# Bit projections in two products instead of three, and bits by comparing two halves

## The chip, the cores and the metric

The kernel runs on one core of a Trainium2 chip. The metric is the device time of one execution in microseconds (us). The kernel is written with explicit semaphores: every engine has its own program, runs it in order and waits where a semaphore says so.

## What is computed

Attention with a bucket mask, then a top-1 mixture of eight experts, then a dense layer pair. The change touches the first part alone, where each query and key gets six bits, one for each column of `proj`; a query may look at a key only if all six agree.

```python
batch, n_heads, seq, head_dim = (2, 8, 768, 64)      # 16 heads; proj is 64 x 6
q_bits = (np.einsum('bhsd,dk->bhsk', q, proj) > 0).astype(np.int64)
k_bits = (np.einsum('bhsd,dk->bhsk', k, proj) > 0).astype(np.int64)
powers = 2 ** np.arange(n_bits)
q_bucket = np.sum(q_bits * powers, axis=-1)
k_bucket = np.sum(k_bits * powers, axis=-1)
mask = q_bucket[:, :, :, None] == k_bucket[:, :, None, :]
scores = scale * np.matmul(q, k.transpose(0, 1, 3, 2))
scores = np.where(mask, scores, -1000000000.0)
...
attn = attn / (np.sum(attn, axis=-1, keepdims=True) + 1e-09)
return np.matmul(attn, v).astype(np.float32)
```

The sign of a projection has to be right for values near zero, so it is not enough to multiply in a reduced format. The kernel splits a number into a high part (rounded to `fp32r`) and a low part (the rest) and adds the products high x high, low weight x high input, and high weight x low input.

## The kernel before

**Stages.** The first 270 us are attention over 16 heads, then come routing (some 15 us), the experts and the dense layers. The experts' stage starts when the last head's rows are written.

**A head.** A head g has two sides, c = 0 (queries) and c = 1 (keys); `u = 2g + c` counts them. Each side holds 768 tokens as 128 partitions x 384 columns: two tokens' 64 dimensions lie above each other, so that partitions 0 to 63 and 64 to 127 hold different tokens. For a side:

- `turn_qk` (TensorE) transposes the raw rows into a bank of PSUM, `bank_a`.
- `split_hi` (ScalarE, lines 595 and 597) copies the bank out as the high part; `split_lo` (VectorE, line 767) makes the low part `x_lo`.
- `project` (TensorE, line 1097) forms three products of 384 columns in the same bank.
- `sign` (VectorE, line 783) makes `bits`, 1.0 where the projection is positive.
- `code` (TensorE, line 1105) multiplies the bits by a pattern matrix, so that all 64 buckets stand in a row each; `mask_even` (VectorE, line 791) and `mask_odd` (ScalarE, lines 605 and 608) turn this into one-hot rows, `q_a` and `k_a`, that the score products add.

GpSimd copies the parts to their places (lines 465 to 496).

**Groups.** The order on each engine is written by hand. A head is three groups (`part` 0, 1, 2), and a group n works on two score tiles of 128 queries. On TensorE a group holds the scores of tiles m_s and m_s + 1 (`pair_s`, `pair_t`, line 1119, eight products), the transposes of earlier exponentials (`turn_exps`, line 1130), and, by part, pieces of an earlier head's product with v (`times_v`, line 1146) and output product (`last`, line 1157), and of the next head's preparation. On VectorE a group holds `copy_t1` (line 799, transposed exponentials out of PSUM) and `row_max` (line 775); on ScalarE `copy_t0` (line 627), `exp_rows` (line 618), `copy_u` (line 634) and `copy_rows`.

**Waits.** Scores of tile m wait for the exp of tile m - 2. `code` waits for `sign`, `turn_qk` of a side waits for both masks of the side before, and `exp_rows` waits for `row_max`. `bank_a` is used by all sides except head 0's keys.

Of the kernel before, what the change touches and what calls it, by code (L numbers as in the profile page):

```python
# [22 lines left out]
ALU = mybir.AluOpType  # L23
ACT = mybir.ActivationFunctionType
AX = mybir.AxisListType
F32 = mybir.dt.float32
F32R = mybir.dt.float32r
# [4 lines left out]
P = 128  # L32
# [4 lines left out]
B, H, S, D = 2, 8, 768, 64  # L37
NBITS = 6
BUCKETS = 2 ** NBITS
HEADS = B * H  # L40
# [15 lines left out]
HALF = S // 2  # L56
# [70 lines left out]
def program(nc, q, k, v, proj, w_gate, w_ogate, w1, w2, w_in, w_out, const, out):  # L127
    with ExitStack() as ctx:
        sem = lambda n: ctx.enter_context(nc.semaphore(n))
# [30 lines left out]
        with ExitStack() as att:  # L160
            sb = lambda n, s, d=F32: att.enter_context(nc.sbuf_tensor(n, s, d))
            sb("w_first", [P, 2, SET])
            v_nat = sb("v_nat", [P, 4, J, D])
            exps = sb("exps", [P, 4, S])
            exps_t = sb("exps_t", [P, J, S])
            den = sb("den", [P, 4, J])
            rows_sb = sb("rows_sb", [P, 2, J, QE])
            u_sb = sb("u_sb", [P, S])
            last_w = sb("last_w", [P, H, QE])
            raw = sb("raw", [P, 2, 2, J, D])  # L170
            q_a = sb("q_a", [P, 2, S], F32R)
            k_a = sb("k_a", [P, 2, S], F32R)
            q_b = sb("q_b", [P, 2, S], F32R)
            k_b = sb("k_b", [P, 2, S], F32R)
            x_lo = sb("x_lo", [P, 2, HALF], F32R)
            bits = sb("bits", [P, 2, HALF], BF16)
            nmax = sb("nmax", [P, 2, J])
            proj2 = sb("proj2", [P, NBITS])
            pat = sb("pat", [P, P])
            pat_bf = sb("pat_bf", [P, P], BF16)  # L180
            proj_w = sb("proj_w", [P, 2, P], F32R)


        with ExitStack() as rt:
# [78 lines left out]
        prep_bank = lambda u: bank_b if u == 1 else bank_a  # L263
# [17 lines left out]
        s_pat = sem("s_pat")  # L281
        s_bits = sem("s_bits")
        s_sgn = sem("s_sgn")
        s_code = sem("s_code")
        s_mq, s_mk = sem("s_mq"), sem("s_mk")
        s_sc = sem("s_sc")
        s_mx = sem("s_mx")
# [300 lines left out]
        def _(act):  # L588
# [10 lines left out]
            def mask_odd(g, c):  # L599
# [7 lines left out]
                else:  # L607
                    act.activation(tiles(k_a, g, 1)[D:P], turned(prep_bank(u))[D:P], ACT.Relu, scale=BIG,
                                   bias=unmatched[D:P, :]).then_inc(s_mk, 1)

            def exp_rows(m):
                g, qt = m // J, m % J
                act.wait_ge(s_mx, m + 1)
                if g >= 4 and qt == 0:
                    act.wait_ge(s_x, g - 3)
                if m >= 4:
                    act.wait_ge(s_pt, 2 * (m - 3))
                act.activation(exps[:, m % 4, :].rearrange("p (h n) -> p h n", h=2), score_pair[m % 2][:, :, 0:HALF],  # L618
                               ACT.Exp, bias=nmax[:, g % 2, qt:qt + 1],
                               accum_out=den[:, g % 4, qt:qt + 1]).then_inc(s_ex, 1)  # L620

            def copy_t0(m):
                g, qt = m // J, m % J
                if g >= 1:
                    act.wait_ge(s_av, 2 * (g - 1) + qt // 3 + 1)
                act.wait_ge(s_pt, 2 * m + 1)
                act.activation(exps_t[:, 0:JH, qt * P:(qt + 1) * P],  # L627
                               pair_u[:, 0, 0:HALF].rearrange("p (j n) -> p j n", j=JH), ACT.Copy).then_inc(s_t0, 1)

            def copy_u(g, h):  # L630
                act.wait_ge(s_av, 2 * g + h + 1)
                if g >= 1:
                    act.wait_ge(s_fin, g)
                act.activation(u_sb[:, h * HALF:(h + 1) * HALF], bank_b[:, 0:HALF], ACT.Copy).then_inc(s_u, 1)  # L634
# [36 lines left out]
            for n in range(3, GROUPS):  # L671
                g, part = n // 3, n % 3
                m_s, m_e = 2 * (n - GROUP_S), 2 * (n - GROUP_E)
                if 0 <= m_e - 1 < J * HEADS - 1:
                    copy_t0(m_e - 1)
                if part == 0 and 3 <= g < HEADS + 2:
                    copy_rows(g - 3)
                if g < HEADS and part == 1:
                    split_hi(g, 1)
                if g < HEADS and part == 2:  # L680
                    mask_odd(g, 1)
                if 0 <= m_e < J * HEADS:
                    copy_t0(m_e)
                if m_s < J * HEADS:
                    exp_rows(m_s)
                    exp_rows(m_s + 1)
                if n == 3 * HEADS + 3:
                    copy_t0(m_e + 1)
                if g >= 2 and part <= 1:
                    copy_u(g - 2, part)  # L690
                if g < HEADS and part == 0:
                    mask_odd(g, 0)
                if g + 1 < HEADS and part == 2:
                    split_hi(g + 1, 0)
# [53 lines left out]
        def _(dve):  # L748
# [11 lines left out]
            def split_lo(g, c):  # L760
                u = 2 * g + c
                if u >= 2:
                    dve.wait_ge(s_cp, copies(u - 2))
                    dve.wait_ge(s_bits, u - 1)
                dve.wait_ge(s_hi, u + 1)
                hi = tiles(k_b, g, 1) if c else tiles(q_b, g, 0)
                dve.scalar_tensor_tensor(turned(x_lo[:, c, :]), turned(prep_bank(u)), SCALE if c else 1.0,
                                         hi.bitcast(F32), ALU.mult, ALU.subtract).then_inc(s_lo, 1)
# [9 lines left out]
            def sign(g, c):  # L778
                u = 2 * g + c
                if u >= 2:  # L780
                    dve.wait_ge(s_code, u - 1)
                dve.wait_ge(s_bits, u + 1)
                dve.tensor_scalar(bits[:, c, :], prep_bank(u)[:, 0:HALF], 0.0, None, ALU.is_gt).then_inc(s_sgn, 1)

            def mask_even(g, c):
                u = 2 * g + c
# [7 lines left out]
            def copy_t1(m):  # L794
                g, qt = m // J, m % J
                if g >= 1:
                    dve.wait_ge(s_av, 2 * (g - 1) + qt // 3 + 1)
                dve.wait_ge(s_pt, 2 * m + 2)
                dve.tensor_copy(exps_t[:, JH:J, qt * P:(qt + 1) * P],  # L799
                                pair_u[:, 1, 0:HALF].rearrange("p (j n) -> p j n", j=JH)).then_inc(s_t1, 1)  # L800
# [23 lines left out]
            for n in range(3, GROUPS):  # L824
                g, part = n // 3, n % 3
                m_s, m_e = 2 * (n - GROUP_S), 2 * (n - GROUP_E)
                if 0 <= m_e - 1 < J * HEADS:
                    copy_t1(m_e - 1)
                if g < HEADS and part == 0:
                    split_lo(g, 0)  # L830
                if m_s < J * HEADS:
                    row_max(m_s)
                if g < HEADS and part == 2:
                    mask_even(g, 1)
                if m_s < J * HEADS:
                    row_max(m_s + 1)
                if g < HEADS and part == 0:
                    sign(g, 0)
                if g < HEADS and part == 1:
                    split_lo(g, 1)  # L840
                if 0 <= m_e < J * HEADS:
                    copy_t1(m_e)
                if g < HEADS and part == 0:
                    mask_even(g, 0)
                if n == 3:
                    dve.wait_ge(s_cst, 16)
                    dve.tensor_copy(last_w[:, :, 0:D],
                                    cc("twice").unsqueeze(1).broadcast_to([P, H, D])).then_inc(s_setup, 1)
                if n == 9:
                    dve.tensor_copy(tri_bf[:, :], cc("tri"))  # L850
                    dve.tensor_copy(ones_bf[:, :], cc("ones"))
                    dve.tensor_copy(iota_bf[:, :], cc("iota"))
                if part == 1 and g >= 2:
                    inverse(g - 2)
                if part == 1 and 8 <= g < 8 + NCH:
                    dve.wait_ge(s_wld[g - 8], 16)
                    dve.tensor_copy(chunk_of(w_part, 0, 0, g - 8), w_raw[0][g - 8][:, :]).then_inc(s_whi, 1)
                if g < HEADS and part == 1:
                    sign(g, 1)
# [216 lines left out]
        def _(pe):  # L1076
# [13 lines left out]
            def project(g, c):  # L1090
                u = 2 * g + c
                hi, lo = (tiles(k_b, g, 1) if c else tiles(q_b, g, 0)), x_lo[:, c, :]
                pe.wait_ge(s_lo, u + 1)
                if u == 0:
                    pe.wait_ge(s_setup, 1)
                for n, (w, x) in enumerate(((0, hi), (1, hi), (0, lo))):
                    mm = pe.matmul(prep_bank(u)[:, 0:HALF], proj_w[:, w, :], x, start=n == 0, stop=n == 2)  # L1097
                mm.then_inc(s_bits, 1)

            def code(g, c):  # L1100
# [293 lines left out]
```

## Time and profile before

| | |
|---|---|
| median of 3 runs | 800.01 us (799.96 to 800.34) |
| profiled execution | 799.7 us |
| its span, first to last instruction | 797.9 us |
| mean granted TensorE clock | 0.999 |
| TensorE (PE) busy | 780.0 us |
| TensorE weight loads (PEld) busy | 657.8 us |
| VectorE (DVE) busy | 454.9 us |
| ScalarE (ACT) busy | 361.7 us |
| GpSimd (POOL) busy | 339.2 us |

The profile is that of one execution. Matmuls are pipelined and their recorded ends are modelled, so the spacing of their starts is a better measure than their length. The chain is followed back from the last instruction, at each step to what released it.

### The profile page before, as it was taken

What the parts mean: (1) busy time and instruction counts of PE and PEld (TensorE: products, weight loads), DVE (VectorE), ACT (ScalarE), POOL (GpSimd) and SP (SyncE); (2) the same over time, 40 slices, a digit from 0 to 9 for tenths busy, and PEclk for the clock granted to TensorE, in tenths of its full rate; (3) what the DMA queues carried; (4) which work ended last, traced back from release to release, by engine and by line L of the source; (5) the groups of instructions that cost most, each with busy time, mean ns of one, the idle gap of its engine ahead of it and who ended that gap; (6) DMA issues with size and microseconds to landing.
All of it is one profiled execution on the core that took longest, in us unless ns stands there. A gap on an engine that the chain in (4) does not pass through costs nothing.

```text
span 797.9 us, 12941 instructions
## 1 busy us (share of the span) xinstructions
PE 780.0 (98%) x4389; PEld 657.8 (82%) x4389; DVE 454.9 (57%) x801; ACT 361.7 (45%) x684; POOL 339.2 (43%) x333
## 2 busy tenths in 40 slices
PE   7999999999999889999999999999999999999997
PEld 5777787778777578888888888899889889989985
DVE  6787778788877574544445445559427416613720
ACT  5777777677766322344322440057117305603610
POOL 4244434565554179977779883125210020000000
PEclk9999999999999999999999999999999999999999
DMA  6222322121100086775656750440010020000000
GB/s 174 80 70 74 101 89 67 50 71 41 41 21 12 21 278 227 248 235 175 196 175 228 239 166 27 155 137 1 26 53 2 1 67 14 0 14 28 1 14 26
DMA packets 40942, 72.68 MB, mean 91 GB/s; under 512 B 17904, under 2 KB 24304, under 8 KB 40880
## 3 DMA queue, kind: packets, MB, share of 16 engines
q10 hardware_dynamic: 9520, 31.60, 12.2%
q1 hardware_dynamic: 27920, 28.98, 11.6%
q0 software_dynamic: 3440, 11.28, 4.3%
q8 instruction: 39, 0.64, 0.3%
q14 instruction: 23, 0.19, 0.1%
HBM read 60.56 MB, written 11.28 MB: 90 GB/s over the span
## 4 chain that ended last, share of the span: by engine, by line
PE 63%; issue 28%; DVE 4%; POOL 2%; ACT 2%; DMA 0%; POOLq 0%; DVEq 0%; ACTq 0%
PE pair_s L1266 13%; PE pair_t L1281 13%; PE bank_b L1146 8%; PE pair_u L1130 8%; PE pair_s L1119 4%; PE pair_t L1119 4%; PE bank_b L1157 2%; PE bank_a L1097 2%; PE pair_u L1245 2%; PE bank_a L1086 1%; POOL out L567 1%; PE pair_s L1318 1%; DVE g_lo L1066 1%; PE bank_a L1105 1%; POOL y_raw L561 1%
## 5 line engine op out<-in xcount | busy, mean ns | idle before, releaser
L436 POOL TENSOR_TENSOR w_part<-w_raw,w_part 128x1024 fp32r<-128x1024 f32 x80 | 190.1, 2405 | 57.5 <-ACT w_part L658 56.8
L658 ACT ACTIVATE w_part<-w_raw 128x1024 fp32r<-128x1024 f32 x72 | 73.9, 1055 | 135.8 <-PE pair_t L1281 102.9
L1368 PE MATMUL pair_t<-w_part,g_hi 128*128 128x512 f32 x384 | 119.0, 391 | 0.3 <-POOL w_part L436 0.3
L1266 PE MATMUL pair_s<-w_part,xs_t 128*128 x456 | 108.8, 394 | 0.4 <-DVE xs_t L944 0.4
L1281 PE MATMUL pair_t<-w_part,hid_t 128*128 x456 | 109.0, 394 | 0.0
L567 POOL DMA_INDIRECT out<-o_sb,token x12 | 11.8, 984 | 208.5 <-DVE o_sb L1036 208.5
L1266 PEld LDWEIGHTS pair_s<-w_part,xs_t 128*128 128x128 f32 x456 | 84.2, 188 | 17.8 <-issue 0.9
L1281 PEld LDWEIGHTS pair_t<-w_part,hid_t 128*128 128x128 f32 x456 | 84.4, 188 | 16.8
L734 ACT ACTIVATE elu<-elu 128x384 f32<-128x384 f32 x64 | 33.6, 524 | 121.2 <-DVE elu L1056 121.1
L1368 PEld LDWEIGHTS pair_t<-w_part,g_hi 128*128 128x128 f32 x384 | 71.6, 188 | 15.2 <-issue 0.7
L1130 PE MATMUL pair_u<-first,exps 128*128 128x128 f32 x576 | 79.2, 273 | 1.5 <-ACT exps_t L627 1.0
L1368 PE MATMUL pair_t<-w_part,g_lo 128*128 128x512 f32 x192 | 74.9, 390 | 0.0
L1130 PEld LDWEIGHTS pair_u<-first,exps 128*128 128x128 f32 x576 | 67.4, 141 | 5.4 <-ACT exps L618 2.0
L1146 PE MATMUL bank_b<-exps_t,v_nat 128*64 128x384 f32 x384 | 69.0, 494 | 0.7 <-ACT u_sb L634 0.7
L1318 PE MATMUL pair_u<-y_t,w_part 128*128 128x384 f32 x384 | 69.3, 334 | 0.3 <-DVE elu L1061 0.3
L1318 PE MATMUL pair_s<-y_t,w_part 128*128 128x384 f32 x384 | 69.3, 335 | 0.0
L1318 PEld LDWEIGHTS pair_u<-y_t,w_part 128*128 128x128 f32 x384 | 66.8, 188 | 0.7 <-DVE elu L1061 0.6
L1318 PEld LDWEIGHTS pair_s<-y_t,w_part 128*128 128x128 f32 x384 | 66.9, 188 | 0.2
L799 DVE COPY exps_t<-pair_u 128x384 f32<-128x384 f32 x96 | 53.1, 553 | 20.4 <-PE pair_u L1130 18.7
L962 DVE CAST hid_t<-pair_u 128x512 fp32r<-128x512 f32 x38 | 26.1, 686 | 67.2 <-PE pair_u L1245 67.2
L627 ACT ACTIVATE exps_t<-pair_u 128x384 f32<-128x384 f32 x96 | 47.2, 491 | 21.0 <-PE pair_u L1130 20.1
L953 DVE TENSOR_SCALAR hid<-pair_s 128x1024 f32<-128x1024 f32 x19 | 23.3, 1225 | 46.8 <-PE pair_s L1266 46.8
(196 smaller groups left out, 1234.9 us busy)
## 6 DMA issues: line engine op xcount, KB each, us to landing
w_raw<-in_moe_w ACTq DMA_DIRECT2D x48, 512.0 KB, 6.2
w_raw<-in_moe_w SPq DMA_DIRECT2D x16, 512.0 KB, 5.0
ys_sorted<-ys SPq DMA_DIRECT2D x19, 256.5 KB, 3.5
w_raw<-in_moe_w_in ACTq DMA_DIRECT2D x8, 512.0 KB, 6.6
raw<-in_q SPq DMA_DIRECT2D x16, 192.0 KB, 2.4
raw<-in_k SPq DMA_DIRECT2D x16, 192.0 KB, 2.6
v_nat<-in_v SPq DMA_DIRECT2D x16, 192.0 KB, 2.3
x_rows<-rows_sb SPq DMA_DIRECT2D x16, 192.0 KB, 2.3
```

The source lines that it names most:

```text
L436: pool.tensor_tensor(chunk_of(w_part, n, 1, c), w_raw[n % 2][c][:, :], chunk_of(w_part, n, 0, c).bitcast(F32), ALU.subtract).then_inc(s_wl ...
L627: act.activation(exps_t[:, 0:JH, qt * P:(qt + 1) * P], pair_u[:, 0, 0:HALF].rearrange("p (j n) -> p j n", j=JH), ACT.Copy).then_inc(s_t0, 1)
L658: act.activation(chunk_of(w_part, n, 0, c), w_raw[n % 2][c][:, :], ACT.Copy).then_inc(s_whi, 1)
L734: act.activation(elu[:, n % 3, :], elu[:, n % 3, :], ACT.Exp).then_inc(s_em, 1)
L799: dve.tensor_copy(exps_t[:, JH:J, qt * P:(qt + 1) * P], pair_u[:, 1, 0:HALF].rearrange("p (j n) -> p j n", j=JH)).then_inc(s_t1, 1)
L1119: mm = pe.matmul(score_pair[m % 2][:, h, 0:HALF], a[:, g % 2, t], b[:, g % 2, h * HALF:(h + 1) * HALF], start=first, stop=not first)
L1130: mm = pe.transpose(pair_u[:, part, n * P:(n + 1) * P], exps[:, m % 4, kt * P:(kt + 1) * P], ident)
L1146: mm = pe.matmul(bank_b[o * D:(o + 1) * D, 0:HALF], v_nat[:, g % 4, 2 * i + o, :], exps_t[:, 2 * i + o, h * HALF:(h + 1) * HALF], start=i ...
L1266: mm = pe.matmul(pair_s[:, h, :], xs_t[:, xp, c * P:(c + 1) * P], w_part[:, bass.ds(par, 1), wp, a:a + 512], start=c == 0 and xp == 0 and ...
L1281: mm = pe.matmul(pair_t[:, s % 2, :], hid_t[:, hp, c * P:(c + 1) * P], w_part[:, bass.ds(par, 1), wp, a:a + DM], start=c == 0 and n == 0, ...
L1318: mm = pe.matmul(hidden_bank[n % 4][:, 0:NB], w_in_p[:, wp, c, f * P:(f + 1) * P], y_t[:, yp, c, :], start=c == 0 and m == 0, stop=c == CD ...
L1368: mm = pe.matmul(pair_t[:, t % 2, :], gp[:, f, j * P:(j + 1) * P], w_out_p[:, wp, f, :], start=f == 0 and m == 0, stop=f == FT - 1 and m == 2)
```

## The change

From head 1 on a side's projection has two products. A third block of the weight operand, `proj_w[:, 2, :]`, has the high weights in columns 0 to 63 and the low weights in columns 64 to 127. One product with the high input gives high x high on the output's partitions 0 to 63 and low x high on 64 to 127; the second product, high weights with the low input, adds to partitions 0 to 63. The projection is the sum of the two halves, which no instruction forms: ScalarE copies the upper half to `low_sb` (`keep_low`), and VectorE writes a bit where minus the lower half is smaller than that copy. Head 0 stays as it was. The third block is built in group 3 by two VectorE copies, and TensorE waits for them at u = 2. `sign` of the query side moves behind `copy_t1` in VectorE's order.

```diff
-            proj_w = sb("proj_w", [P, 2, P], F32R)
+            proj_w = sb("proj_w", [P, 3, P], F32R)
+            low_sb = sb("low_sb", [P, 2, HALF])
...
+            def keep_low(g, c):
+                u = 2 * g + c
+                act.wait_ge(s_sgn, u - 1)
+                act.wait_ge(s_bits, u + 1)
+                act.activation(low_sb[0:D, c, :], prep_bank(u)[D:P, 0:HALF], ACT.Copy).then_inc(s_low, 1)
...
                 if 0 <= m_e < J * HEADS:
                     copy_t0(m_e)
+                if g < HEADS and part == 0:
+                    keep_low(g, 0)
                 if m_s < J * HEADS:
                     exp_rows(m_s)
                     exp_rows(m_s + 1)
...
                 if g >= 2 and part <= 1:
                     copy_u(g - 2, part)
+                if g < HEADS and part == 1:
+                    keep_low(g, 1)
...
-                dve.wait_ge(s_bits, u + 1)
-                dve.tensor_scalar(bits[:, c, :], prep_bank(u)[:, 0:HALF], 0.0, None, ALU.is_gt).then_inc(s_sgn, 1)
+                if g == 0:
+                    dve.wait_ge(s_bits, u + 1)
+                    dve.tensor_scalar(bits[:, c, :], prep_bank(u)[:, 0:HALF], 0.0, None, ALU.is_gt).then_inc(s_sgn, 1)
+                else:
+                    dve.wait_ge(s_low, u - 1)
+                    dve.scalar_tensor_tensor(bits[0:D, c, :], prep_bank(u)[0:D, 0:HALF], -1.0, low_sb[0:D, c, :],
+                                             ALU.mult, ALU.is_lt).then_inc(s_sgn, 1)
...
+                if n == 3:
+                    dve.wait_ge(s_setup, 1)
+                    for w in range(2):
+                        done = dve.tensor_copy(proj_w[:, 2, w * D:(w + 1) * D], proj_w[:, w, 0:D].bitcast(F32))
+                    done.then_inc(s_both, 1)
...
-                if g < HEADS and part == 0:
-                    sign(g, 0)
                 if g < HEADS and part == 1:
                     split_lo(g, 1)
                 if 0 <= m_e < J * HEADS:
                     copy_t1(m_e)
+                if g < HEADS and part == 0:
+                    sign(g, 0)
...
-                for n, (w, x) in enumerate(((0, hi), (1, hi), (0, lo))):
-                    mm = pe.matmul(prep_bank(u)[:, 0:HALF], proj_w[:, w, :], x, start=n == 0, stop=n == 2)
+                if u == 2:
+                    pe.wait_ge(s_both, 1)
+                parts = ((0, hi), (1, hi), (0, lo)) if g == 0 else ((2, hi), (0, lo))
+                for n, (w, x) in enumerate(parts):
+                    mm = pe.matmul(prep_bank(u)[:, 0:HALF], proj_w[:, w, :], x, start=n == 0, stop=n == len(parts) - 1)
```

On VectorE the query side of a steady head stood so before; `bits` is `sign`, `q_a` is `mask_even`, and the second row of `exps_t` belongs to the next group:

```order
L767 SCALAR_TENSOR_TENSOR x_lo<-bank_a,q_b 128x384
L775 TENSOR_REDUCE nmax<-pair_s 128x1
L775 TENSOR_REDUCE nmax<-pair_t 128x1
L783 TENSOR_SCALAR bits<-bank_a 128x384
L799 COPY exps_t<-pair_u 128x3x128
L791 TENSOR_SCALAR q_a<-bank_a,first 64x3x128
L799 COPY exps_t<-pair_u 128x3x128
```

And so in the changed kernel, with its own line numbers:

```order
L780 SCALAR_TENSOR_TENSOR x_lo<-bank_a,q_b 128x384
L788 TENSOR_REDUCE nmax<-pair_s 128x1
L788 TENSOR_REDUCE nmax<-pair_t 128x1
L817 COPY exps_t<-pair_u 128x3x128
L800 SCALAR_TENSOR_TENSOR bits<-bank_a,low_sb 64x384
L809 TENSOR_SCALAR q_a<-bank_a,first 64x3x128
L817 COPY exps_t<-pair_u 128x3x128
```

`sign` changed places with `copy_t1` and has a second operand. On ScalarE, the same stretch and the next group before; `u_sb` is `copy_u`, `rows_sb` is `copy_rows`:

```order
L642 ACTIVATE rows_sb<-bank_b 128x480
L627 ACTIVATE exps_t<-pair_u 128x3x128
L618 ACTIVATE exps,den<-pair_s,nmax 128x768
L618 ACTIVATE exps,den<-pair_t,nmax 128x768
L634 ACTIVATE u_sb<-bank_b 128x384
L605 ACTIVATE q_a<-bank_a,first 64x3x128
L627 ACTIVATE exps_t<-pair_u 128x3x128
L597 ACTIVATE k_b<-bank_a 128x3x128
L627 ACTIVATE exps_t<-pair_u 128x3x128
L618 ACTIVATE exps,den<-pair_s,nmax 128x768
L618 ACTIVATE exps,den<-pair_t,nmax 128x768
L634 ACTIVATE u_sb<-bank_b 128x384
```

And in the changed kernel:

```order
L651 ACTIVATE rows_sb<-bank_b 128x480
L636 ACTIVATE exps_t<-pair_u 128x3x128
L618 ACTIVATE low_sb<-bank_a 64x384
L627 ACTIVATE exps,den<-pair_s,nmax 128x768
L627 ACTIVATE exps,den<-pair_t,nmax 128x768
L643 ACTIVATE u_sb<-bank_b 128x384
L608 ACTIVATE q_a<-bank_a,first 64x3x128
L636 ACTIVATE exps_t<-pair_u 128x3x128
L600 ACTIVATE k_b<-bank_a 128x3x128
L636 ACTIVATE exps_t<-pair_u 128x3x128
L627 ACTIVATE exps,den<-pair_s,nmax 128x768
L627 ACTIVATE exps,den<-pair_t,nmax 128x768
```

One copy to `low_sb` stands ahead of the two exps of part 0; the one of the key side comes behind the `u_sb` of part 1, one row further on.

## Rows read from the trace of the kernel before

**Rows 1.** The page, part 1: busy time of each engine.
```profile
PE 780.0 (98%) x4389; PEld 657.8 (82%) x4389; DVE 454.9 (57%) x801; ACT 361.7 (45%) x684; POOL 339.2 (43%) x333
```

**Rows 2.** Windows, attention stage: PE, PEld, DVE, ACT, POOL busy, clock, DMA.
```profile
20.00:260.00 240.00, 239.31 (x1643) 188.33 (x1642) 187.64 (x309) 173.51 (x373) 112.16 (x188) 1.00 0.21 60
```

**Rows 3.** Chain that ended last, one head: start, us, what.
```profile
119.55 0.70 PE pair_s L1119 x4
...
121.60 0.53 PE bank_a L1097 x3
...
124.22 0.27 PE bank_a L1105
...
125.14 0.70 PE pair_s L1119 x4
...
129.63 0.73 PE bank_a L1097 x3
...
132.43 0.18 PE bank_a L1105
...
135.55 0.70 PE pair_s L1119 x4
```

**Rows 4.** Groups by form on TensorE, 23 to 246 us: busy, mean ns.
```profile
L1097 PE MATMUL bank_a<-x_lo,proj_w 128*128 128x384 f32 x28 | 9.4, 337 | 0.0
```

**Rows 5.** Timeline of ScalarE, the same head: start, us.
```profile
121.76 0.90 ACT L618 ACTIVATE exps<-pair_s,nmax 128x768 f32<-128x768 f32 x1
...
122.64 0.90 ACT L618 ACTIVATE exps<-pair_t,nmax 128x768 f32<-128x768 f32 x1
...
124.26 0.49 ACT L634 ACTIVATE u_sb<-bank_b 128x384 f32<-128x384 f32 x1 [0.64 <-PE bank_b L1146]
124.78 0.57 ACT L605 ACTIVATE q_a<-bank_a,first 64x384 fp32r<-64x384 f32 x1
...
129.68 0.49 ACT L634 ACTIVATE u_sb<-bank_b 128x384 f32<-128x384 f32 x1
130.79 0.49 ACT L627 ACTIVATE exps_t<-pair_u 128x384 f32<-128x384 f32 x1 [0.62 <-PE pair_u L1130]
...
134.71 0.89 ACT L618 ACTIVATE exps<-pair_t,nmax 128x768 f32<-128x768 f32 x1
```

**Rows 6.** Timeline of VectorE, the same head.
```profile
120.21 0.56 DVE L767 SCALAR_TENSOR_TENSOR x_lo<-bank_a,q_b 128x384 fp32r<-128x384 f32 x1
...
121.55 0.95 DVE L775 TENSOR_REDUCE nmax<-pair_t 128x1 f32<-128x768 f32 x1
122.42 0.55 DVE L783 TENSOR_SCALAR bits<-bank_a 128x384 bf16<-128x384 f32 x1
122.88 0.55 DVE L799 COPY exps_t<-pair_u 128x384 f32<-128x384 f32 x1
...
130.47 0.56 DVE L783 TENSOR_SCALAR bits<-bank_a 128x384 bf16<-128x384 f32 x1 [0.66 <-PE bank_a L1097]
...
133.39 0.96 DVE L775 TENSOR_REDUCE nmax<-pair_t 128x1 f32<-128x768 f32 x1
```

**Rows 7.** Timeline of TensorE at the start; in brackets idle time and releaser.
```profile
14.10 0.34 PE L1105 MATMUL bank_a<-bits,pat_bf 128*128 128x384 bf16 x1 [1.41 <-DVE bits L783]
...
17.80 0.63 PE L1097 MATMUL bank_a<-k_b,proj_w 128*128 128x384 f32 x2 [0.88 <-DVE x_lo L767]
...
21.70 0.52 PE L1086 MATMUL bank_a<-first,raw 128*128 128x128 f32 x3 [0.21 <-DVE k_a L791]
```

**Rows 8.** Timeline of VectorE at the start.
```profile
13.50 0.55 DVE L783 TENSOR_SCALAR bits<-bank_a 128x384 bf16<-128x384 f32 x1
...
18.71 0.56 DVE L783 TENSOR_SCALAR bits<-bank_a 128x384 bf16<-128x384 f32 x1 [0.50 <-PE bank_a L1097]
...
20.98 0.61 DVE L791 TENSOR_SCALAR k_a<-bank_a,first 64x384 fp32r<-64x384 f32 x1
```

**Rows 9.** Timeline of ScalarE at the start, the fourth exp's accumulator.
```profile
18.87 0.20 ACT L618 ACTIVATION_READ_ACCUMULATOR exps<-pair_t,nmax 128x1 f32 x1
```

More of the change, by code:

```diff
@@ L283, in program @@
         s_sgn = sem("s_sgn")
+        s_low = sem("s_low")
         s_code = sem("s_code")
+        s_both = sem("s_both")
         s_mq, s_mk = sem("s_mq"), sem("s_mk")
```

## The prediction

> **What bounds the kernel now.** I read the page first, then the windows, then the chain, then the timelines of the engines around the edit, and last the first 24 us, where the edit also puts new waits.
>
> On the page the reader is to see TensorE busy for 98% of the span [rows 1]. Busy time of pipelined matmuls can flatter, so the windows come next: in the 240 us from 20 to 260, the attention stage, TensorE has 239.31 us, at a granted clock of 1.00, its upper level of 2.4 GHz [rows 2]. The decisive view is the chain that ended last [rows 3]. Through one head it holds nothing but TensorE pieces, one behind another: scores at 119.55 and again at 135.55 are the same place in two neighbouring heads, so a head costs 16.00 us. So in the steady heads an instruction taken off TensorE is worth its full spacing, until something else comes late. The attention stage is followed by routing and the experts, which start when the last head is done, so what is won there is handed on.
>
> **The change, part by part.**
>
> *The removed product.* A projection of head 1 or later has two products instead of three. The chain gives three products in 0.53 us for the q side [rows 3], 0.177 each. The k side takes 0.73, the same three plus 0.20 ahead of the first one, which follows the 64-column products of times_v; that 0.20 stays, since a first product stays. There are 28 such projections between 23 and 246 us, that is 14 heads with two sides each: the 28 `x_lo` products of [rows 4], one for each. 28 x 0.176 = 4.9 us, if nothing comes late.
>
> The Trainium skill, page "TensorE: Matmul & The Clock Gate", section "Back-to-back issue gap", gives a warm isolated gap of N/2.4 + 2.5 ns, an estimate of 162.5 ns at 384 columns, by which the removed products would be worth 4.55 us. The row shows 177 and has this kernel's weight loads in it, so I stay with the row; the two differ by 0.4 us.
>
> *keep_low, the q side (steady heads).* ScalarE gets a 64x384 copy out of PSUM. No row of before is that instruction. Its nearest rows are the 128x384 copy out of PSUM, 0.49 us, and the 64x384 form with a bias, 0.57 [rows 5]; I take 0.49. When can it start? The products of head g's q side end at 122.13 by the chain (121.60 + 0.53), 0.18 earlier now: 121.95. A hand-over from TensorE costs about 0.1 (the k side ends at 129.63 + 0.73 = 130.36 [rows 3], and VectorE's bits start at 130.47 [rows 6]). So keep_low runs from 122.05 to 122.54. Behind it on ScalarE stand the two exps, which started at 121.76 and 122.64 [rows 5]: they move to about 122.5 and 123.4 and end by 124.4. Who waits for them? The scores of the next group at 125.14 on TensorE (124.96 now) [rows 3] want the first, which is done by 123.5; those 0.70 behind them want the second, done by 124.4 against 125.7. The ScalarE copy u_sb, at 124.26 [rows 5], starts at about 124.4, and its reader is the times_v of the next group, which stands behind eight score products and two turns. ScalarE then stands idle until TensorE has turned the next k side, where the 0.75 us is made up. So this costs nothing; its cover is ScalarE's waiting for TensorE before u_sb (0.64 us in [rows 5]) and over 1 us of slack at the next scores.
>
> *sign, the q side.* It moves behind copy_t1 on VectorE and becomes a scalar_tensor_tensor. The priced neighbour is x_lo, the same form from the same bank, 0.56 [rows 6], against 0.55 for the old one. VectorE's queue goes 121.55 row_max, 122.42 copy_t1, 122.88 sign, the last two having changed places [rows 6], and low_sb is there at 122.6, so the queue decides and not ScalarE. The bits are ready at 123.44. TensorE wants them for code at 124.22 [rows 3], 124.04 now. Slack 0.6 us, where there was 1.25. Cost nothing; were the chain of two engines later by x, each head would pay x - 0.6.
>
> *keep_low and sign, the k side.* The products end at 130.36 - 0.35 = 130.01. ScalarE has just finished u_sb (129.68 [rows 5], 0.18 earlier now) and used to stand idle 0.62 us before the copy at 130.79. keep_low fits in this hole: 130.12 to 130.61. VectorE's sign then runs from 130.66 to 131.21, and code wants it at 132.43 - 0.35 = 132.08 [rows 3]: slack 0.87. Against TensorE's new pace the VectorE queue behind it is some 0.35 us late, shrinking to 0.15 to 0.25 at the second row_max, which was at 133.39 and ended at 134.35 [rows 6], 0.36 before its exp at 134.71 [rows 5]. That is the thinnest margin of the steady heads: used up, but not crossed.
>
> *The start, head 1.* Here TensorE isn't full and waits for VectorE, so the same edits cost. Two 128x64 copies build the third weight part ahead of the first row_max: nothing to 0.46 us each (the spacing of 128x384 copies in [rows 6]); I take 0.25 for both, since they have a sixth of the elements each. The bits at 13.50 and TensorE's code at 14.10, which already waited 1.41 us, move by that 0.25 [rows 7, 8], so does the k side at 17.80, which waits for x_lo; it then saves 0.18. Next, head 1's k side: keep_low stands behind two exps on ScalarE, and the second's accumulator read ends at 19.07 [rows 9], 19.3 now. keep_low runs to 19.75, sign starts at 19.8 instead of 18.71 [rows 8]. Behind sign on VectorE come copy_t1 (20.26), row_max (20.72) and mask_even of k_a at 21.6, which was at 20.98 [rows 8]. For that one TensorE already waited, at 21.70 [rows 7]: it now starts at about 22.3. After this TensorE is full again. So head 1 costs +0.6 us with its two removed products already in it. Bounds: -0.35 (all hidden) and +1.1 (sign's whole lateness).
>
> The larger memset at the start lies in VectorE's first idle wait. The s_both wait is over when scores end.
>
> *The sum.* -4.9 + 0.6 = -4.3 us on the profiled execution of 799.7 (span 797.9 and 1.8 around it): 795.4. The median is 0.3 above that execution: **795.7 us**.
>
> **The rivals.**
>
> *A, new waits eat part of it.* The margins of 0.6 (q side) and 0.36 (second exp) are crossed by some tenths, for instance because a PSUM copy that starts at partition 64 and lands at 0, or the compare with an SBUF operand, is dearer than its neighbours. For it: the path now goes over two engines and two hand-overs. Against: it takes 0.6 before anything is paid. At 0.1 us a head, 14 heads give back 1.4: 797.1.
>
> *B, slower.* The mechanism is code of the q side, waiting on TensorE for sign, behind keep_low. It decides when the chain keep_low to sign is more than 0.6 + 0.35 = 0.95 us longer than worked out; at 1.2 us longer a head pays 0.6 and saves 0.35, so 14 x 0.25 + 0.6 = +4.1: 804. No row has a copy of this size above 0.6 us, so little speaks for it.
>
> *C, no change.* TensorE isn't what bounds the stage, and the removed product turns into idle time. Weight loads are busy only 188.33 of 240 us [rows 2]. Against: the chain has no piece of another engine between 119.55 and 135.55. In that case the time is 800 to 800.6 with the start's loss. The Trainium skill, page "Trainium Kernel Development and Optimization", section "Best Practices", says to judge the distance to the roofline by the weight loads' busy share and not by the matmuls'; by that 78% this stage would have room, and the rule speaks for C. It concerns the distance to the peak, while the chain tells who waits for whom, and I follow the chain.
>
> *D, the start costs nothing.* Then -4.9 - 0.35: 794.8. It is a variant of the forecast.
>
> That the edit doesn't do what it says is excluded by the instruction order: each later projection has two products.
>
> **How the numbers follow.** Forecast, D with it (794.6 to 796.6): 0.80. A (796.6 to 798.4): 0.08. C: 0.08. B: 0.04. The range reaches from D's end a little into A: 794.5 to 797.2. About 0.2%, 1.6 us, is what a measurement of this kernel tells from no change; forecast and A lie below 798.4, so faster 0.88, same 0.08, slower 0.04.
>
> **What would show it.** In the changed profile: 66 projection products where there were 96; a head of 15.65 us in the chain, still TensorE alone; ScalarE copies of 0.49; sign at 0.56 starting right behind copy_t1 on the q side; no wait of TensorE for bits in the steady heads; a wait of some 0.8 us before the first turn of head 2. The forecast is wrong if the chain shows VectorE or ScalarE pieces once a head, or if a head is shorter by much other than 0.35.

## The result

The changed kernel takes 797.95 us, median of 15 runs (797.57 to 798.88), against 799.96 us (15 runs) for the kernel before: a ratio of 0.9977, 95% interval 0.997 to 0.9984. It is 2.0 us faster; 4.3 us were forecast, and the range (794.5 to 797.2) does not hold the median. In 8 of the 15 runs the mean granted clock was 0.998 or more and the time 797.57 to 797.95; in the other 7 it was 0.995 to 0.997 and the time 798.24 to 798.88. The profiled execution is one of the 7: it took 798.58 us, with a span of 796.7 us and a mean granted clock of 0.996 where before had 0.999.

From the page, busy time of each engine, to be held against [rows 1]; 30 products and 30 weight loads fewer, 30 ScalarE copies more:

```profile
PE 778.7 (98%) x4359; PEld 654.1 (82%) x4359; DVE 451.5 (57%) x803; ACT 376.7 (47%) x714; POOL 338.9 (43%) x333
```

The chain of the changed kernel over one steady head (start, us, what), against [rows 3]:

```profile
119.62 0.33 PE bank_a L1109 x3
119.95 0.74 PE pair_u L1156 x6
...
122.76 0.35 PE bank_a L1123 x2
...
130.61 0.56 PE bank_a L1123 x2
...
135.36 0.33 PE bank_a L1109 x3
```

It is still TensorE alone, and both projections lost their product (0.53 to 0.35, 0.73 to 0.56). But the turns of the next head's query side (`bank_a L1109`), 15.74 us apart, say that a head takes 15.74 and not 15.65. The one piece that grew by more than 0.02 is the six transposes behind the turn (`pair_u L1156`): 0.74 us, where all other groups of six take 0.65 or 0.66.

Then the start. Windows of TensorE in the changed kernel: stretch, its length, busy (matmuls), granted clock, DMA share, GB/s:

```profile
10.00:15.00 5.00, 3.06 (x16) 1.00 0.41 119
15.00:20.00 5.00, 4.95 (x24) 0.66 0.21 62
```

And the timeline of TensorE there:

```profile
14.45 0.34 PE L1131 MATMUL bank_a<-bits,pat_bf 128*128 128x384 bf16 x1 [1.51 <-POOL q_b L497]
14.69 0.59 PE L1145 MATMUL pair_s<-k_a,q_a 128*128 128x384 f32 x2
15.11 0.56 PE L1145 MATMUL pair_s<-k_b,q_b 128*128 128x384 f32 x2
15.57 0.98 PE L1145 MATMUL pair_t<-k_a,q_a 128*128 128x384 f32 x2
16.35 0.84 PE L1145 MATMUL pair_t<-k_b,q_b 128*128 128x384 f32 x2
```

From about 15.4 to 18.8 us the clock was granted at its lower level, 1.2 GHz: two products that take 0.51 at 2.4 GHz take 0.84. The kernel before kept 1.00 in these windows. This fall is in the profiled execution, but not in each (below).

Two stretches of each trace hold nearly the whole account; what comes after them took 527.05 us before and 526.84 changed. The first goes from head 1's query turn to head 2's query turn (10.12 to 21.70 in the kernel before, 10.26 to 24.14 in the changed one), the second from there to the first product after the last head (270.83 and 269.89).

| | start, us | second stretch, us |
|---|---|---|
| before | 11.58 | 249.13 |
| changed | 13.88 (+2.30) | 245.75 (-3.38) |
| forecast | +0.6 | -4.9 |

### The profile page after: what moved, and what is told of

Same layout as the page of the kernel before. It is cut to its first block, busy times and chain, and to the rows that moved or that the text cites. A ratio compares the mean times of both kernels' runs of the same rounds, so it can differ in the third digit from the quotient of the medians.

```text
span 796.7 us, 12944 instructions
## 1 busy us (share of the span) xinstructions
PE 778.7 (98%) x4359; PEld 654.1 (82%) x4359; DVE 451.5 (57%) x803; ACT 376.7 (47%) x714; POOL 338.9 (43%) x333
## 4 chain that ended last, share of the span: by engine, by line
PE 62%; issue 28%; DVE 4%; POOL 3%; ACT 2%; DMA 0%; POOLq 0%; DVEq 0%; ACTq 0%
PE pair_s L1292 13%; PE pair_t L1307 13%; PE bank_b L1172 8%; PE pair_u L1156 7%; PE pair_t L1145 4%; PE pair_s L1145 4%; PE pair_u L1271 2%; PE bank_b L1183 2%; PE bank_a L1123 2%; PE bank_a L1109 1%; POOL out L570 1%; PE pair_s L1344 1%; DVE g_lo L1089 1%; PE bank_a L1131 1%; POOL y_raw L564 1%
## 5 line engine op out<-in xcount | busy, mean ns | idle before, releaser
L1156 PE MATMUL pair_u<-first,exps 128*128 128x128 f32 x576 | 81.0, 276 | 1.8 <-ACT exps_t L636 1.0
L1156 PEld LDWEIGHTS pair_u<-first,exps 128*128 128x128 f32 x576 | 67.8, 142 | 7.1 <-ACT exps L627 2.0
```

Of the source, the lines that this page charges most:

```text
L1156: mm = pe.transpose(pair_u[:, part, n * P:(n + 1) * P], exps[:, m % 4, kt * P:(kt + 1) * P], ident)
```

## The experiments

Theory after the result: (1) the removed products are worth what was forecast, (2) in a steady head the last `copy_t1` of part 2 reaches TensorE late, because the key side's bits now pass over ScalarE, (3) head 1 loses more than forecast, and on top of it the clock may fall. The rivals stand in the expectations. All times are medians. A start is the first stretch above, and its difference is against before's 11.58; a difference of a second stretch is against 249.13. The kernel before was 799.78, 799.78 and 799.80 in the three sets of runs.

**New bits, old products.**

```diff
-                parts = ((0, hi), (1, hi), (0, lo)) if g == 0 else ((2, hi), (0, lo))
+                parts = ((0, hi), (1, hi), (0, lo))
```

> The changed kernel with the old three products in every head; the keep_low copy and the comparison stay. Its upper output half is zero, so the bits are the same. Theory: in a steady head the last copy_t1 of part 2 reaches TensorE's transposes 0.09 us late, because ScalarE's and VectorE's work for the key side starts when the projection ends; that distance does not depend on how many products there were, so the head takes 16.00 + 0.09 = 16.09 us and the kernel is slower than before, by 14 x 0.09 = 1.3 plus what head 1 costs (0.6 to 2.8): 801.9 to 804. Rival, that the steady loss only comes about because TensorE is now faster than VectorE's queue: a head of 16.00 us and no TensorE wait there.

Measured: 802.24 us, ratio 1.0031 (1.0019 to 1.0043). Start 12.78 (+1.20), second stretch 250.45 (+1.32), a steady head 16.05 to 16.07 where before has 15.99. All six executions have a mean clock of 0.998 or more. From its chain:

```profile
104.81 0.74 PE pair_u L1156 x6
...
106.96 0.66 PE pair_u L1156 x6
```

The same transposes take 0.74 although TensorE has its three products. So the loss belongs to the new path of the bits and not to TensorE having become faster; the rival falls. The new path by itself costs 2.5 us.

**Two products, old bits.** No `keep_low`, and `sign` as before, with its single operand and in its old place (the diff shows the operand alone). The bits then leave out the product of the low weights, so this kernel computes less than the reference:

```diff
-                    dve.scalar_tensor_tensor(bits[0:D, c, :], prep_bank(u)[0:D, 0:HALF], -1.0, low_sb[0:D, c, :],
-                                             ALU.mult, ALU.is_lt).then_inc(s_sgn, 1)
+                dve.tensor_scalar(bits[:, c, :], prep_bank(u)[:, 0:HALF], 0.0, None, ALU.is_gt).then_inc(s_sgn, 1)
```

> Two products, but the old single-operand sign in its old place and no keep_low. The bits then leave out the product of the low weights, so part of the computation is left out. Theory: with no third engine in the path nothing comes late: a steady head of 15.65 us, no half clock at the start, time -4.9 -0.35 +0.3 (the two copies): 795. Rival, that the missing product itself (less work for TensorE at the start) brings the half clock: granted clock below 1 between 15 and 19 us and 796.5 to 797.

Measured: 794.97 us, ratio 0.9943 (0.9929 to 0.9957). Start 11.59 (+0.01), second stretch 244.22 (-4.91), a steady head 15.61. Its chain:

```profile
117.26 0.66 PE pair_u L1147 x6
...
132.87 0.66 PE pair_u L1147 x6
```

The transposes are back at 0.66. The products are worth 4.9 us here, as forecast, though not in the way forecast (see below). Three executions took 794.82 to 794.97; the other two took 795.38 and 796.03 with a mean clock of 0.996 and 0.997. The profile is of one of the three and has a clock of 1.00 at the start; where the clock of the two fell, no trace shows. So this run does not exclude its rival, that the missing product is what lets the clock fall.

**Fillers in the hole at the start.**

```diff
+                if n == 3:
+                    for _ in range(8):
+                        pe.matmul(bank_b[:, 0:HALF], pat_bf[:, :], bits[:, 1, :], start=True, stop=True)
                 if g < HEADS and part == 0:
                     code(g, 0)
```

> The changed kernel with eight extra products of 384 columns into an idle bank, between the projection and the code of head 1's query side, where TensorE stood idle 1.5 us. They add nothing to the output. Theory: the half clock from 15.4 to 18.8 us comes from TensorE's idle time ahead of it, and it costs 1 to 1.8 us; with the hole filled the clock stays at 1.00 and the time is 796.3 to 797. Rival, the start's loss is the waits of head 1 alone: the same 798.

Measured: 797.36 us (797.18 to 797.46 in six runs), ratio 0.9969 (0.9957 to 0.9981). Start 12.62, second stretch 245.63. The clock:

```profile
10.00:15.00 5.00, 4.38 (x24) 1.00 0.39 119
15.00:20.00 5.00, 4.35 (x30) 1.00 0.42 112
```

No execution had a mean clock below 0.998. But 12.62 is still 1.04 above before: this is what head 1's waits cost without the clock, and the clock's fall is the other 1.26 of the 2.30. The two ends of that cost, on ScalarE and on TensorE:

```profile
19.67 0.49 ACT L618 ACTIVATE low_sb<-bank_a 64x384 f32<-64x384 f32 x1
...
22.89 0.52 PE L1109 MATMUL bank_a<-first,raw 128*128 128x128 f32 x3 [1.01 <-DVE k_a L809]
```

**Head 1 by the old path**, with `g <= 1` in place of `g == 0` in the projection and in `sign`, no `keep_low` for head 1, and TensorE's wait for the two copies moved to u = 4:

```diff
-                parts = ((0, hi), (1, hi), (0, lo)) if g == 0 else ((2, hi), (0, lo))
+                parts = ((0, hi), (1, hi), (0, lo)) if g <= 1 else ((2, hi), (0, lo))
```

> Head 1 goes by the old path too (three products, single-operand sign, no keep_low); only heads 2 to 15 are changed, the two weight copies stay in group 3. Theory: the start then loses only the 0.2 of the copies, the clock mostly holds, and the steady heads give 14 x 0.26 = 3.6: 796.4 to 796.8. Rival, that the half clock comes from the copies alone: clock below 1 near 15 us and about 797.5 to 798.

Measured: 796.57 us (796.43 to 797.04), ratio 0.9959 (0.9946 to 0.9973). Start 11.77 (+0.19), second stretch 245.69 (-3.44), clock 1.00 throughout the start, although TensorE's idle stretch there is 1.61 us, longer than the changed kernel's 1.51. Undoing the change in one head of fifteen makes it 1.4 us faster than the whole change.

**The two copies alone**, added to the kernel before:

> The kernel before with one thing added: the two 128x64 weight copies on VectorE in group 3 and TensorE's wait for them; nothing uses them. Theory: they hold up head 1's bits and code by 0.2 us, which is passed on as TensorE waits there: 0.2 us slower, 800.0 to 800.2, clock 1.00 from 10 to 25 us. Rival, that the copies alone bring the half clock: granted clock below 1 near 15 us and over 801.

Measured: 800.22 us, ratio 1.0002 (0.9993 to 1.0011), and this chip scattered more than the others (before: 798.51 to 801.28). Its trace tells more than its time: start 11.77, exactly the +0.19 of the run above, clock 1.00; no execution has a mean clock below 0.998. The copies alone don't bring the fall. Its second stretch is 249.43 (+0.30): the stretch from head 3's query turn to head 4's takes 16.23 us where before has 15.95, for the mask of k_a that the open points below tell of.

**sign behind the copy.** The key side's `sign(g, 1)` moved from the end of part 1 to behind the first `copy_t1` of part 2:

> The changed kernel with the key side's sign moved behind the next copy_t1 on VectorE, for all heads. Theory: VectorE stands idle before this sign, so copy_t1 fills the hole and the queue behind it comes 0.1 us earlier; the last copy_t1 of part 2 is then in time for TensorE and a steady head takes 15.61 to 15.66 instead of 15.74: 1.1 to 1.8 us faster than the changed kernel in the same state of the clock, 796 to 797. Rival, that sign itself is now late for code: a TensorE wait in front of code and a head of 15.74 or more.

Measured: 797.94 us, ratio 0.9982 (0.9973 to 0.9991). The theory of this run fell: a steady head takes 15.79, more than the changed kernel's 15.74, and the piece that grew is again the transposes behind the turn, from 0.74 to 0.81. The start takes 12.17, less than with the fillers, and the second stretch 246.55, so the second loses more than the first gains; 5 of its 11 executions have a mean clock of 0.996 or 0.997. VectorE's timeline:

```profile
114.93 0.56 DVE L817 COPY exps_t<-pair_u 128x384 f32<-128x384 f32 x1 [1.98 <-PE pair_u L1156]
115.40 0.54 DVE L800 SCALAR_TENSOR_TENSOR bits<-bank_a,low_sb 64x384 bf16<-64x384 f32 x1
```

There is no hole for the copy to fill, since its own input, TensorE's transposes after the projection, is ready no earlier than `low_sb` was. The queue starts 1.31 us after the projection's start (113.62 in the chain) instead of 1.24.

**Fillers in the kernel before.**

> The kernel before with the eight extra 384-column products in group 3, where it stands idle 1.4 us. Theory: before does not lose its clock there in most executions, so they change nothing: 799.8 to 800.1. Rival, that the fillers help by themselves, whatever the clock, or are dear: 799.0 or less, or above 800.5.

Measured: 799.88 us, ratio 0.9998 (0.9989 to 1.0007), start 11.58: nothing, as expected. Two of its 11 executions have a mean clock of 0.996 and 0.997 (800.29 and 801.45 us), so fillers in this hole don't keep the clock up in every execution of every kernel.

**Head 1 old, copies in group 4, sign behind the copy.**

> Heads 2 to 15 as changed, head 1 by the old path, the two weight copies in group 4 where VectorE waited, and from head 2 on the key side's sign behind the next copy_t1. Theory: nothing is lost at the start and a steady head takes 15.61 to 15.66, so 14 x 0.34 to 0.39 = 4.8 to 5.5 us less than before: 794.4 to 795.2. Rival, that the steady waits are only moved: as with head 1 alone undone, 796.5.

Measured: 796.98 us, ratio 0.9968 (0.9956 to 0.998), on the scattering chip. Start 11.58, nothing lost; a steady head about 15.79 again, for the reason above. Half of its theory held.

**copy_t1 before the second row_max** in part 2, heads 2 to 15:

```diff
+                late = part == 2 and 2 <= g < HEADS
-                if m_s < J * HEADS:
+                if m_s < J * HEADS and not late:
                     row_max(m_s + 1)
...
                     copy_t1(m_e)
+                if late:
+                    row_max(m_s + 1)
```

> The changed kernel with one swap on VectorE from head 2 on: in part 2 the last copy_t1 stands before the second row_max. Theory: the steady loss is this copy reaching TensorE's transposes late, behind a queue that begins with the key side's sign; one row_max (0.87 us) further forward it is in time, and a steady head takes 15.61 to 15.66 us, 1 to 1.8 us less in all than the changed kernel of this call. Rival: the second row_max, now 0.5 us later, makes its exp late for the next scores, TensorE waits in front of pair_t in part 0, and a head takes 15.74 or more.

Measured: 799.25 us, ratio 0.9994 (0.9985 to 1.0003), with four of 11 executions at 800.00 to 800.42 and a mean clock of 0.997 or 0.998. The rival it is: the transposes are in time, and the scores wait instead. Chain, then ScalarE's timeline:

```profile
119.29 0.66 PE pair_u L1159 x6
119.95 0.70 PE pair_s L1148 x4
120.65 0.89 PE pair_t L1148 x4
```

```profile
119.46 0.91 ACT L627 ACTIVATE exps<-pair_t,nmax 128x768 f32<-128x768 f32 x1 [0.24 <-DVE nmax L788]
```

0.66 where the changed kernel has 0.74, but 0.89 where it has 0.69 to 0.72; a head takes 15.85. The test does show that this copy was what the transposes waited for. Up to and with head 1 this kernel is the changed one, and its trace gives the counterpart to the fall: TensorE's holes are the same, the clock stays.

```profile
14.48 0.34 PE L1134 MATMUL bank_a<-bits,pat_bf 128*128 128x384 bf16 x1 [1.51 <-POOL q_b L497]
...
15.15 0.51 PE L1148 MATMUL pair_s<-k_b,q_b 128*128 128x384 f32 x2
15.61 0.59 PE L1148 MATMUL pair_t<-k_a,q_a 128*128 128x384 f32 x2
```

Its start takes 12.62, as with the fillers.

**The same swap with head 1 old and the copies in group 4.**

> Heads 2 to 15 as changed with the same swap of copy_t1 and row_max, head 1 by the old path, the two weight copies in group 4. Theory: the losses add up and both are gone, -14 x 0.35 to 0.39 = -4.9 to -5.4 against the kernel before: 794.4 to 794.9. Rival, the swap gives nothing: the same as the next kernel of this call.

Measured: 798.00 us, ratio 0.9977 (0.9968 to 0.9986). The theory fell with the one before: start 11.57, but 247.38 in the second stretch.

**Head 1 old and the copies in group 4, no swap.** The two copies stand at n == 4, behind `copy_t1`:

> Head 1 by the old path and the two weight copies in group 4, heads 2 to 15 as changed, no swap. Theory: against the kernel before nothing is lost at the start, and the steady heads give 14 x 0.26, less about 0.2 in head 3: -3.4 to -3.7, 796.2 to 796.5; 0.2 less than with the copies in group 3. Rival, that the copies' place is of no account: 796.6.

Measured: 796.38 us (796.15 to 796.46), ratio 0.9957 (0.9943 to 0.997). Start 11.56, nothing lost; second stretch 245.57 (-3.56); a steady head 15.71. This is the fastest kernel of the study that computes all of the reference, 3.4 us under before.

**The changed kernel again.**

> The changed kernel once more, on the chip of this call. Theory: executions fall into two groups, those in which the clock falls to half near 15 us (798.5 to 798.9) and those in which it does not (797.6 to 798.0). Rival, one group around 798.0, so that the half clock of the profiled execution says nothing of the time.

Measured: 798.41 us, ratio 0.9976 (0.9967 to 0.9985), and two groups: 798.41 to 798.94 in the six executions whose mean granted clock is 0.996, 797.47 to 797.81 in the five with 0.998 or more. A profile with the fall (start 13.94) belongs to the first. So the slower group is about 1 us above the other and holds about half of the executions; only two executions of it, the two profiled ones, show that the clock fell at the start.

## Why the prediction was wrong

**The removed product: right in kind, and the total partly by luck.** 28 x 0.176 = 4.9 was forecast, and with nothing in its way -4.91 was measured. But a steady head lost 0.38 (15.99 to 15.61) for two products, 0.19 each and not 0.176, which over 14 heads would be 5.3. The stretch from head 3's query turn to head 4's gained only 0.03 (15.95 to 15.92), because VectorE's mask of k_a was late once (see the open points), and so the sum came back to 4.9. The Trainium skill, page "TensorE: Matmul & The Clock Gate", section "Back-to-back issue gap", gives the isolated gap that the prediction worked out as 162.5 ns; this trace's 0.19 us lies above it.

**TensorE bounds the stage: right**, so rival C is out. The Trainium skill, page "Trainium Kernel Development and Optimization", section "Best Practices", whose rule on the weight loads' busy share spoke for it, concerns the distance to the roofline; here weight loads were busy 78% of the stage while each product taken off shortened a steady head in full.

**keep_low and sign, the q side: right.** The copy takes 0.49, `sign` stands right behind `copy_t1` (123.47, 123.94) and code does not wait.

**keep_low and sign, the k side: wrong, and this is the largest part.** The step said that the VectorE queue is late against TensorE's new pace, by 0.15 to 0.25 at the second row_max, and called its exp "the thinnest margin". The lateness was right, and that exp is in time. But behind the second row_max stands one more instruction that the prediction did not follow to what waits for it, the last `copy_t1`. VectorE in the changed kernel:

```profile
131.85 0.55 DVE L800 SCALAR_TENSOR_TENSOR bits<-bank_a,low_sb 64x384 bf16<-64x384 f32 x1 [1.06 <-ACT low_sb L618]
...
134.40 0.96 DVE L788 TENSOR_REDUCE nmax<-pair_t 128x1 f32<-128x768 f32 x1
135.28 0.55 DVE L817 COPY exps_t<-pair_u 128x384 f32<-128x384 f32 x1
```

It ends at 135.83. It reads half of `pair_u`, and the second half of TensorE's next six transposes overwrites that half, so they wait for it; and what has to wait is not their product but the weight load ahead of it. The weight loads of the changed kernel (from the first, and from the fourth on):

```profile
135.42 0.77 PEld L1156 LDWEIGHTS pair_u<-first,exps 128*128 128x128 f32 x6
...
135.88 0.31 PEld L1156 LDWEIGHTS pair_u<-first,exps 128*128 128x128 f32 x3
```

And of the kernel before, with its copy:

```profile
118.27 0.55 DVE L799 COPY exps_t<-pair_u 128x384 f32<-128x384 f32 x1
...
118.63 0.69 PEld L1130 LDWEIGHTS pair_u<-first,exps 128*128 128x128 f32 x6
```

The loads start 0.11 us apart, so the fourth is due 0.33 us after the first, at 135.75. The copy ends at 135.83, and the load starts at 135.88. In the kernel before the load was due at 118.96 and the copy ended at 118.82. So the margin was 0.14 us, much thinner than the 0.36 that was taken for the thinnest; the copy is 0.22 later against TensorE, and 0.08 of this crosses the margin. A head gives back 0.08 of its gain for it. Against the head without the new path (15.61) it is 0.13 in all; the other 0.05 lies in pieces that are up to 0.02 longer each (the key side's projection takes 0.56 for 0.54), and its cause was not followed. The second stretch gives back 4.91 - 3.38 = 1.5 us. The prediction said that it would be wrong if the chain showed VectorE pieces once a head, or if a head was shorter by much other than 0.35: the second sign came (0.25), the first did not, since a wait this short stands inside TensorE's own piece. Rival A had this form (new waits eat part of it), with the wrong places and a chance of 0.08.

**The start: the mechanism right, its size wrong.** +0.6 was forecast for head 1 and +1.04 measured without the fall of the clock. The same chain ran as described: exps, `low_sb`, sign, copy, row_max, k_a, turn. Its beginning was mis-sized. With the fillers `low_sb` starts at 19.67, 0.27 later than the forecast's 19.25, once the 0.15 by which that whole start is later are taken off. The exps ahead of it moved by 0.42 and not by the 0.25 of the copies, because `keep_low` of the query side stands ahead of the exps of the group before, too, for which scores wait. ScalarE's hand-over to VectorE took 0.10 where 0.05 was taken, and the mask of k_a starts 0.97 behind its row_max where 0.88 was taken. The two copies cost 0.19; 0.25 was taken. "The s_both wait is over when scores end" was wrong: TensorE stood 0.17 us in front of head 1's first projection for the copies.

**The clock: missing.** The prediction took the clock of 1.00 as given. Idle stretches of 0.17 and 1.51 us on TensorE were followed by the fall in the profiled execution (0.16 and 1.51 in the second profile), and not in that of the kernel with `copy_t1` moved, which is the same up to there. The kernel before, with an idle stretch of 1.41 us, took more than 801 us in 2 of 15 executions. With the 1.51 us filled, none of six executions has a mean clock below 0.998. What is shown is that fillers and head 1's old path remove the slower group; what decides was not found. It is not the longest idle stretch alone, which was 1.61 us with head 1 old. Nor is it the new path of the bits alone: with it and three products no execution of six has a lower mean clock, while with two products and the old bits two of five have. This points at the missing products, but with so few executions, and none of those two traced, it is not shown. The Trainium skill, page "TensorE: Matmul & The Clock Gate", section "Why this matters for your kernels", says to avoid idle gaps over about 3 us; here the longest idle stretch in the 5 us ahead of the fall was 1.51 us, so keeping to this advice was not enough.

**The sum.** +1.04 - 3.38 = -2.3 gives 797.6, the faster group; the fall adds 0.9 to 1.3 in about half of the executions: 798.6. The median of 797.95 is the slowest run of the faster group, and all of that group lies above the range's end of 797.2. So the forecast fails without the clock: of the 2.0 us between -4.3 and -2.3, 1.5 are the late `copy_t1` and the new path in the steady heads, put at nothing, and 0.4 the mis-sized start.

What stays open: in every kernel but the one before, with and without fillers, VectorE once, at 37 to 40 us, starts its mask of k_a late, by 0.14 to 0.43 us, with no engine named as the cause. The `copy_t1` behind it is then late for TensorE's transposes. This is worth up to 0.3 us once. It comes with the two copies alone as well, so the new path of the bits is not needed for it; it was not pursued. Also open is how to give VectorE its 0.1 us back in the steady head: both reorderings only moved the wait.

## What to carry to other kernels

When an instruction moves later on an in-order engine, follow every instruction behind it to whatever waits for it, until the queue is idle again, and not only up to the thinnest margin found so far. On TensorE the due time is that of the weight load: here it starts 0.11 us ahead of its product's record, and 0.27 us ahead of the piece in the chain. A chain that names one engine alone does not show that its margins hold: compare each piece with its like. A change that is repeated over all heads pays per head in the steady part, and pays differently in the pipeline's fill, where no engine hides it: leaving head 1 on the old path was worth 1.4 us of 800 by the medians, and 0.85 us of it by the starts of traces without the clock's fall (12.62 and 11.77). Where a start has holes on TensorE, look at the granted clock of many executions, not of one.

## What the hardware showed that was not expected

The changed kernel's executions fall into two groups by mean granted clock. Two programs that are alike up to there, with the same holes on TensorE (0.17 and 1.51 us), ran one execution with the clock at its lower level from 15.4 to 18.8 us and another at the upper level.

A wait stands in front of the weight load, ahead of the product: the fourth load of the transposes starts at 135.88, 0.05 us after the end of the copy it waits for and 0.13 later than due, while products before it still run.

A hand-over from ScalarE to VectorE took 0.10 us (`low_sb` ended at 131.75, sign started at 131.85), like one from TensorE (by the chain its products ended at 131.16, `low_sb` started at 131.26).
